# Attention on one Trainium2 core: the last 64 rows of q and k turned together, their scores by one tile over the whole array

## What is computed

```python
scores = scale * np.matmul(q, k.transpose(0, 1, 3, 2))          # scale = 1/8
cum = np.cumsum(np.maximum(s, 0.0), axis=-1)
bias = -(cum[:, :, :, None] - cum[:, :, None, :])
scores = np.where(causal, -1000000000.0, scores + np.minimum(bias, 0.0))
scores = scores - np.max(scores, axis=-1, keepdims=True)
attn = np.exp(scores); attn = attn / (np.sum(attn, axis=-1, keepdims=True) + 1e-09)
out = np.matmul(attn, v)
```

## Time and profile before

| what | value |
|---|---|
| median of 3 runs | 814.59 us (811.77 to 815.05) |
| profiled execution, its own time | 806.68 us |
| its span, first to last instruction | 804.9 us |
| TensorE matmul busy | 748.0 us (93%) |
| VectorE busy | 454.2 us (56%) |
| ScalarE busy | 284.5 us (35%) |
| GpSimd busy | 384.5 us (48%) |
| mean granted TensorE clock | 0.968 |
| attention, last product of TensorE | ends at about 223.4 us |

### The profile page before, as it was taken

The page is one execution under the profiler, slowest core; times in us unless marked ns, Lnnn a source line. Parts: engine busy times, 40 slices in busy tenths (PEclk is TensorE's granted clock), DMA queues, the critical chain, the costliest instruction groups (busy, mean ns, idle before and its releaser), DMA issues.

```text
span 804.9 us, 14992 instructions
## 1 busy us (share of the span) xinstructions
PE 748.0 (93%) x4920; PEld 613.1 (76%) x4920; DVE 454.2 (56%) x1018; ACT 284.5 (35%) x575; POOL 384.5 (48%) x468
## 2 busy tenths in 40 slices
PE   5999999999946999999999999998497999999998
PEld 2667777776735888888888888886397989979786
DVE  3667767667675444543544544443389962947800
ACT  3667776777520013111121221100154531524401
POOL 6557777777407549744444944400543521313300
PEclk9999999999966999999999999999598999999999
DMA  7787877766133575434433543000401111010011
GB/s 178 179 215 199 221 198 193 215 163 165 44 121 105 155 243 192 146 144 172 145 139 118 208 158 118 27 14 27 131 28 32 41 46 40 1 40 14 11 56 52
DMA packets 98055, 94.43 MB, mean 117 GB/s; under 512 B 62124, under 2 KB 71876, under 8 KB 97988
## 3 DMA queue, kind: packets, MB, share of 16 engines
q1 hardware_dynamic: 79748, 47.87, 21.7%
q10 hardware_dynamic: 14768, 34.38, 12.0%
q0 software_dynamic: 3472, 11.28, 4.7%
HBM read 77.44 MB, written 16.06 MB: 116 GB/s over the span
## 4 chain that ended last, share of the span: by engine, by line
PE 70%; DVE 14%; DMA 6%; POOL 4%; issue 3%; ACT 2%; SPq 1%; POOLq 0%; DVEq 0%; ACTq 0%
PE row_bank L1127 14%; PE wide_bank L1114 14%; PE row_bank L1306 8%; PE turn_ps L298 6%; PE score_ps L270 5%; DVE conv L1353 5%; PE turn_ps L395 5%; DMA x_slots<-x_rows,token_of 5%; PE wide_bank L1294 4%; DVE conv L1351 3%; PE turn_ps L356 3%; PE score_ps L264 2%; POOL ring L832 2%; PE wide_bank L1138 2%; PE turn_ps L275 2%
## 5 line engine op out<-in xcount | busy, mean ns | idle before, releaser
L832 POOL TENSOR_TENSOR ring<-raw_w,ring 128x2048 fp32r<-128x2048 f32 x30 | 137.7, 4613 | 85.7 <-ACT ring L822 85.7
L1114 PE MATMUL wide_bank<-ring,xs_tr 128*128 x600 | 145.8, 399 | 2.8 <-DVE xs_tr L1165 2.6
L1127 PE MATMUL row_bank<-ring,h_tr 128*128 x600 | 143.3, 394 | 1.9 <-DVE h_tr L1185 1.9
L822 ACT ACTIVATE ring<-raw_w 128x2048 fp32r<-128x2048 f32 x30 | 55.8, 1907 | 223.7 <-DMA raw_w<-in_moe_w_dram 194.4
L1114 PEld LDWEIGHTS wide_bank<-ring,xs_tr 128*128 128x128 f32 x600 | 112.9, 191 | 26.5 <-issue 3.7
L1127 PEld LDWEIGHTS row_bank<-ring,h_tr 128*128 128x128 f32 x600 | 110.9, 188 | 24.8 <-issue 2.1
L1294 PE MATMUL wide_bank<-x_tr,ring 128*128 128x288 f32 x768 | 109.8, 303 | 1.3 <-DVE x_tr L1327 1.3
L1294 PEld LDWEIGHTS wide_bank<-x_tr,ring 128*128 128x128 f32 x768 | 106.1, 194 | 2.1 <-DVE x_tr L1327 1.7
L1268 POOL TENSOR_TENSOR conv<-h_pad,conv 128x576 f32<-128x576 f32 x32 | 48.1, 1505 | 122.1 <-ACT conv L1378 122.0
L1306 PE MATMUL row_bank<-ring,g_tr 128*128 128x512 f32 x432 | 99.3, 390 | 3.0 <-ACT out_sb L1410 3.0
L1306 PEld LDWEIGHTS row_bank<-ring,g_tr 128*128 128x128 f32 x432 | 80.7, 188 | 20.7 <-DVE g_tr L1334 4.2
(11 more groups left out here) (176 smaller groups left out, 981.2 us busy)
## 6 DMA issues: line engine op xcount, KB each, us to landing
raw_w<-in_moe_w_dram ACTq DMA_DIRECT2D x12, 2048.0 KB, 10.1
ncum_row<-cum_rows SPq DMA_DIRECT2D x15, 576.0 KB, 4.1
y_sorted<-y_sb SPq DMA_DIRECT2D x25, 256.0 KB, 2.7
raw_w<-in_moe_w_dram SPq DMA_DIRECT2D x12, 512.0 KB, 3.9
ncum_tail<-cum_rows SPq DMA_DIRECT2D x32, 144.0 KB, 4.4
out_dram<-out_sb ACTq DMA_DIRECT2D x18, 256.0 KB, 2.0
q_nat<-in_q_dram SPq DMA_DIRECT2D x32, 128.0 KB, 3.9
v_nat<-in_v_dram SPq DMA_DIRECT2D x32, 128.0 KB, 2.4
```

Of the source, the lines that this page charges most:

```text
L832: nc.gpsimd.tensor_tensor(low, whole, high.bitcast(F32), ALU.subtract).then_inc(low_ready, 1)
L1114: last = nc.tensor.matmul(h_bank[:, half, :], xs_tr[:, a, kb, :], ring[:, bass.ds(n, 1), b, at:at + FH].rearrange("p a c -> p (a c)"), sta ...
L1127: last = nc.tensor.matmul(y_bank[:, :], h_tr[:, a, kb, :], ring[:, bass.ds(n, 1), 2 + b, kb * D:(kb + 1) * D].rearrange("p a c -> p (a c)" ...
```

## The change

`k_nat` loses its tail block; the k tail is loaded to partitions 64 to 127 of the tail block of `q_nat`, under the q tail. One transpose of the whole 128 x 128 tile then gives the turned q tail in 64 columns and the turned k tail in the next 64. `q_tail` becomes a tile of 128 x 128: its first 64 columns hold the q tail of the first head on that head's partitions and zeros elsewhere, its last 64 columns the same for the second head. VectorE writes it by one multiplication of the turned q tail, read twice, with a constant tile `own_head` (the scale on a head's own partitions, zero on the other's), which four memsets fill at the start. The tail scores are then two products (one for each half of the columns) of this tile with all 128 partitions of `k_tr`.

```diff
--- before.py
+++ after.py
@@ -53,7 +53,8 @@
     v_nat = [sb(f"v_nat{u}", [P, NT, 2 * D]) for u in range(2)]
     q_tr = [sb(f"q_tr{u}", [P, BODY]) for u in range(2)]
     k_tr = [sb(f"k_tr{u}", [P, S]) for u in range(2)]
-    q_tail = [sb(f"q_tail{u}", [P, TAIL]) for u in range(2)]
+    q_tail = [sb(f"q_tail{u}", [P, 2, TAIL]) for u in range(2)]
+    own_head = sb("own_head", [P, 2, TAIL])
     ncum_row = [sb(f"ncum_row{u}", [P, 2, S]) for u in range(2)]
     ncum_tail = [sb(f"ncum_tail{u}", [P, S]) for u in range(2)]
     ncum_diag_tail = sb("ncum_diag_tail", [P, TAIL])
@@ -74,7 +75,7 @@
     mask = sb("mask", [P, P])
     mask_tail = sb("mask_tail", [P, TAIL])
     q_nat = [sb(f"q_nat{u}", [P, NT, 2 * D]) for u in range(2)]
-    k_nat = [sb(f"k_nat{u}", [P, NT, 2 * D]) for u in range(2)]
+    k_nat = [sb(f"k_nat{u}", [P, FULL, 2 * D]) for u in range(2)]
 
     def over(name, shape, tensor):
         return nc.alloc_sbuf_tensor_at(name, shape, F32, offset=nc.lookup_mls(tensor).memorylocations[0].addr)
@@ -85,7 +86,7 @@
     score_ps = [ps(f"score_ps{n}", [P, 2, 512]) for n in range(2)]
     turn_ps = [ps(f"turn_ps{n}", [P, 512]) for n in range(4)]
 
-    consts_ready, masks_ready, zeros_ready = sem("consts_ready"), sem("masks_ready"), sem("zeros_ready")
+    consts_ready, masks_ready, zeros_ready, heads_ready = sem("consts_ready"), sem("masks_ready"), sem("zeros_ready"), sem("heads_ready")
     s_loaded, s_clipped, cum_ready, cum_stored = sem("s_loaded"), sem("s_clipped"), sem("cum_ready"), sem("cum_stored")
     col_turned, col_ready = sem("col_turned"), sem("col_ready")
     qk_loaded = [sem(f"qk_loaded{u}") for u in range(2)]
@@ -118,17 +119,17 @@
         return turn_ps[(13 * p + use) % 4]
 
     def sync_part(sp, early, between):
-        def load(dst, src, p, done, tail=0):
+        def load(dst, src, p, done, tail=0, tail_dst=None):
             heads = src[2 * p:2 * p + 2, :, :]
             for hh in range(2):
                 sp.dma_start(dst[:, 0:FULL, hh * D:hh * D + D], src[2 * p + hh, 0:BODY, :].rearrange("(i p) d -> p i d", p=P)).then_inc(done, 16)
-            sp.dma_start(dst[tail:tail + TAIL, FULL, :].rearrange("p (h d) -> p h d", h=2),
+            sp.dma_start((dst if tail_dst is None else tail_dst)[tail:tail + TAIL, FULL, :].rearrange("p (h d) -> p h d", h=2),
                          heads[:, BODY:S, :].rearrange("h p d -> p h d")).then_inc(done, 16)
 
         def load_qk(p):
             above(sp, k_turned, p - 1)
             load(q_nat[p % 2], q_h, p, qk_loaded[p % 2])
-            load(k_nat[p % 2], k_h, p, qk_loaded[p % 2])
+            load(k_nat[p % 2], k_h, p, qk_loaded[p % 2], tail=P - TAIL, tail_dst=q_nat[p % 2])
 
         def load_v(p):
             above(sp, pv_done, NT * (p - 1))
@@ -259,10 +260,8 @@
             above(pe, score_ready, unit(p, n - 2) if i else unit(p, 0) - 1)
             if i == FULL:
                 for half in range(2):
-                    for hh in range(2):
-                        at, rows = slice(hh * D, hh * D + D), slice(hh * TAIL, (hh + 1) * TAIL)
-                        last = nc.tensor.matmul(out[rows, half, 0:HALF], q_tail[u][at, :], k_tr[u][at, half * HALF:(half + 1) * HALF],
-                                                start=True, stop=True)
+                    last = nc.tensor.matmul(out[:, half, 0:HALF], q_tail[u][:, :, :].rearrange("p h c -> p (h c)"),
+                                            k_tr[u][:, half * HALF:(half + 1) * HALF], start=True, stop=True)
                 last.then_inc(scored, 1)
                 return
             for hh in range(2):
@@ -284,9 +283,7 @@
 
         def turn_qk_tails(p):
             u, bank = p % 2, turn(p - 1, 2)
-            nc.tensor.transpose(bank[:, 3 * P:3 * P + TAIL], q_nat[u][0:TAIL, FULL, :], identity[0:TAIL, 0:TAIL])
-            nc.tensor.transpose(bank[:, 3 * P + TAIL:4 * P], k_nat[u][0:TAIL, FULL, :], identity[0:TAIL, 0:TAIL])\
-                .then_inc(tails_turned, 1)
+            nc.tensor.transpose(bank[:, 3 * P:4 * P], q_nat[u][:, FULL, :], identity[:, :]).then_inc(tails_turned, 1)
 
         def turn_k(p):
             above(pe, out_moved, 2 * (p - 2) + 1)
@@ -472,6 +469,8 @@
         for hh in range(2):
             rows = slice(hh * TAIL, (hh + 1) * TAIL)
             nc.vector.tensor_copy(mask_tail[rows, :], mask[rows, rows]).then_inc(masks_ready, 1)
+            nc.vector.memset(own_head[rows, hh, :], SCALE)
+            nc.vector.memset(own_head[rows, 1 - hh, :], 0.0).then_inc(heads_ready, 1)
         dve.wait_ge(col_turned, 1)
         nc.vector.tensor_copy(cum_col[:, :, :], turn_ps[2][:, 0:FULL * HEADS].rearrange("p (i h) -> p i h", h=HEADS))\
             .then_inc(col_ready, 1)
@@ -513,7 +512,8 @@
         def move_qk_tails(p):
             u = p % 2
             dve.wait_ge(tails_turned, p + 1)
-            nc.vector.tensor_scalar(q_tail[u][:, :], turn(p - 1, 2)[:, 3 * P:3 * P + TAIL], SCALE, None, ALU.mult)
+            nc.vector.tensor_tensor(q_tail[u][:, :, :], turn(p - 1, 2)[:, 3 * P:3 * P + TAIL].unsqueeze(1).to_broadcast([P, 2, TAIL]),
+                                    own_head[:, :, :], ALU.mult)
             nc.vector.tensor_copy(k_tr[u][:, BODY:S], turn(p - 1, 2)[:, 3 * P + TAIL:4 * P]).then_inc(tails_moved, 1)
 
         def move_k(p):
@@ -584,6 +584,7 @@
 
         early(dve)
         dve.wait_ge(zeros_ready, 1)
+        dve.wait_ge(heads_ready, 2)
         move_qk_tails(0)
         move_k(0)
         add_bias(0, 0)
@@ -672,7 +673,7 @@
 
         for hh in range(2):
             act.dma_start(k_nat[0][:, 0:FULL, hh * D:hh * D + D], k_h[hh, 0:BODY, :].rearrange("(i p) d -> p i d", p=P)).then_inc(qk_loaded[0], 16)
-        act.dma_start(k_nat[0][0:TAIL, FULL, :].rearrange("p (h d) -> p h d", h=2), k_h[0:2, BODY:S, :].rearrange("h p d -> p h d"))\
+        act.dma_start(q_nat[0][P - TAIL:P, FULL, :].rearrange("p (h d) -> p h d", h=2), k_h[0:2, BODY:S, :].rearrange("h p d -> p h d"))\
             .then_inc(qk_loaded[0], 16)
         act.wait_ge(consts_ready, 4)
         nc.scalar.activation(gates[:, :, 0:P], identity[:, :].unsqueeze(1).to_broadcast([P, PER_B, P]), ACT.Copy).then_inc(gates_loaded, 1)
```

## The result

| | before | after |
|---|---|---|
| median, the runs of the result | 814.8 us (811.8 to 815.5, 4 runs) | 804.0 us (803.0 to 804.3, 4 runs) |
| ratio, 95% interval | | 0.987 (0.985 to 0.990) |
| profiled execution, own time / span | 806.7 / 804.9 us | 803.0 / 801.2 us |
| period of a pair | 12.85 us | 12.39 us |
| start of attention's last product | 221.83 us | 215.46 us |

What follows compares the result with a forecast made beforehand. TensorE was taken to bound attention. Tail scores (4.35 us) and turning the tails (2.31 us) sum to 6.7 us, so 814.6 - 6.7 = 807.9 us; range 805 to 811 within the forecast, 804 to 812.3 overall.

Steps and rivals of the forecast that it cites:

- attention's 6.7 us: Attention: tail scores save 15 x 0.29 = 4.35 us, turning the tails 14 x 0.165 = 2.31 us.
- TensorE bounds attention, and a pair's saving counts each time: Attention: TensorE is always busy, so its saving shortens every pair, the period going from 12.85 to 12.39 us.
- A change of shape costs 0.14 to 0.15 us, at two ends: TensorE in attention: entering the 128*128 shape costs 0.05 us extra, leaving it 0.09 us.
- Rival 3: Tail scores: the gaps belong to something else and return, so they save nothing; 812.3 us, chance 0.07.
- The whole-array slot goes by columns, 0.24 us: Tail scores: four whole-array slots of 288 columns take 0.24 us each, as the four slots before did.
- Rival 2: Tail scores: each pass waits for its own 0.19 us weight load; 4.8 us slower, 819.4 us, chance 0.03.
- The start doesn't gain: Attention's start: savings before 28.42 us only lengthen TensorE's 0.26 us wait for the k load of pair 2.
- VectorE hides the longer move: VectorE in attention: the multiplication takes 0.29 us, 0.08 more, hidden by 0.62 us idle ahead of L506.
- Rival 1: Attention: TensorE's freed time becomes a wait for ScalarE or VectorE, only turning the tails gains; 812.3 us, chance 0.08.
- The median: Whole kernel: the profiled execution's saving applies equally to the 814.6 us median, giving 807.9 us.
- the noise: Experts' start: when the clock rises can shift, for 1 or 2 us either way in both kernels.

Runs made afterwards that it cites:

- e2: Changed kernel with only the block-diagonal tail scores, tails loaded and turned as in the kernel before: 810.0 us, ratio 0.997 to the kernel before.
- e3: Changed kernel with only the tails' joined load and transpose, tail scores as in the kernel before: 812.6 us, ratio 1.000 to the kernel before.
- e8: Changed kernel with the two small 128*64 products moved next to the products with v: 801.5 us, ratio 0.986 to the kernel before.
- e5: Changed kernel with the tail scores in six products of 96 columns instead of two of 288: 813.0 us, one execution.
- e7: Changed kernel with SyncE's five small loads issued behind the loads of pair 2 instead of ahead: 799.1 us, one execution.
- e11: Changed kernel with the edits of e7, e8 and e9 together: 799.8 us, ratio 0.986 to the kernel before.
- e13: Changed kernel with the edits of e7 and e9, without that of e8: 798.9 us, ratio 0.986 to the kernel before.
- e12: Changed kernel with two more 128x512 sums on VectorE right behind the new multiplication: 799.4 us, one execution.
- e4: Changed kernel run again without an edit: 805.1 us, ratio 0.993 to the kernel before.
- e10: Changed kernel run again without an edit, on another chip than e4: 804.7 us, ratio 0.993 to the kernel before.
- e1: Kernel before, run again without an edit for a second trace: 814.4 us, beside 810.9 us in other runs of the same code.
- e9: Changed kernel with GpSimd's splitting of the third expert's weights put among the 25 gathers instead of behind them: 802.8 us, beside 804.7 unedited.

## Why the prediction was right

Direction and range held, the range by luck: the median of 804.02 us lies at its very end, 804. What the prediction worked out is attention's 6.7 us, and this was 6.4 by the logits' start; counted from the transposes of pair 2 on (28.42 and 28.69), it is 6.64. By its steps:

- **TensorE bounds attention, and a pair's saving counts each time.** Shown: the period went to the 12.39 us that was worked out, with no pair off it.
- **A change of shape costs 0.14 to 0.15 us, at two ends.** Shown by e2 (0.30 for two), e3 (0.16 for one and a little array time), and e8, where two more went from other instructions. Rival 3 (it doesn't do what it says) is out.
- **The whole-array slot goes by columns, 0.24 us.** Shown: four slots in 0.97. Rival 2 (loads in the open) is out at this length, and e5 shows from where a load decides: slots under 0.109 us. The 0.19 us that the rival took for a load is too much for one that follows another.
- **The start doesn't gain.** Right, and by 0.27 us worse in this trace, through a later landing, which differs by more than that between executions. That load, not TensorE, sets the start: with it issued first (e7, e11, e13) the wait is gone, and the transposes start at 27.40 to 27.79.
- **VectorE hides the longer move.** Right: the multiplication took 0.27 us (0.29 forecast). But I had looked for its cover at the wrong place. The idle time before L505 is 0.33, which is 0.62 - 0.29 with nothing taken off for the multiplication: that came out of the idle time before L500. By e12 the cover is at least 1.26 us, where the two idle times make 1.05: here they were a lower bound of the cover, not the cover.
- **Rival 1 (the freed time becomes a wait)** didn't come about for this change, and did for the next one of its kind, e8.
- **The median.** I took 814.6 as where the kernel before stands. Its timed executions on five occasions (84, with the outliers 818.9 and 822.9 left out: 805.7 to 817.9) have a median of 811.9, those of the changed kernel on three (28, 799.7 to 811.3) one of 804.3; the fastest are 6.0 us apart. The interval of the result (8 to 12.5 us) leaves the forecast out, those of e4 and e10 (about 2.5 to 9 us) hold it. So the 10.8 us of the result are 6.4 us of attention, and beyond that the draw: three of the four executions of the kernel before were long ones. The term that was mis-sized is the noise, put at 1 or 2 us. Its main source in the traces is the wait for the third expert's weights, 0 to 5.3 us, with the clock's dip behind it (1.6 us more in e1, 2.4 in e10), and I had not looked for what sets it, though the 7.9 us between the profiled execution and the median called for it. That the long executions of untraced runs are of the same kind is likely, and only argued; e9 and e13, where they are missing, speak for it.
- **The 2.6 us given back.** TensorE's timeline near the end of the experts, in the first trace before and in the first after:

```profile
556.27 5.73 PE L1127 MATMUL row_bank<-ring,h_tr 128*128 x24 [1.91 <-DVE h_tr L1185]
569.11 1.09 PE L1276 MATMUL bank<-identity,y_tok 128*128 128x128 f32 x4 [7.11 <-DVE y_tok L1321]
```

```profile
550.10 7.37 PE L1128 MATMUL row_bank<-ring,h_tr 128*128 x24 [1.92 <-DVE h_tr L1186]
564.62 1.08 PE L1277 MATMUL bank<-identity,y_tok 128*128 128x128 f32 x4 [7.15 <-DVE y_tok L1322]
```

The changed kernel is 6.2 us ahead at the first of these rows, 4.5 at the second, 4.0 at 587 us and 3.7 at the end: the run of 24 records took 1.6 us longer. The stage around it, each kernel in its own time (columns of the earlier trace rows), before, after, and in e1, which is the kernel before:

```profile
545.00:565.00 20.00, 15.09 (x70) 12.06 (x68) 5.15 (x8) 0.00 (x0) 0.00 (x0) 1.00 0.08 27
```

```profile
540.00:560.00 20.00, 15.56 (x65) 12.23 (x63) 4.47 (x7) 0.00 (x0) 0.00 (x0) 0.91 0.07 27
```

```profile
550.00:570.00 20.00, 16.20 (x68) 12.83 (x66) 5.03 (x8) 0.00 (x0) 0.00 (x0) 0.91 0.04 15
```

The clock dips to 0.91 in the trace after and not in the one before; but it does so in e1 too, where nothing was changed. So most of what was given back is a dip that the kernel before has as well in some executions. Of the changed kernel's traces e4 and e10 have it too, and among its variants e7, e8, e12 and e13 don't; which executions have it is open. The other 1 us is not accounted for.

## What to carry to other kernels

Read TensorE's timeline from start to start, with the shape of the tile beside each run, and solve for the slot and for what is left over at each change of shape. Where small products stand among whole-array ones, a block-diagonal tile that keeps the shape can be cheaper than concurrent small tiles, although half of it multiplies zeros. Prove such a small gain by the period in the trace and not by medians, which differed by 3.5 us for one and the same code. And where a profiled execution and the median of the runs lie apart, look for a wait that some executions draw and others don't, before anything is forecast in us.

## What the runs showed of the hardware

- On 128*128 tiles, in float32, at a granted clock of 1.00, a slot is the longer of two: 0.109 us for a load of 128 columns (e5), and the columns streamed, 0.24 us for 288.
- A change of tile shape cost 0.09 us ahead of the new shape's first record and 0.05 us in its first slot, the same to 0.01 or 0.02 us for 64*128, 128*64 and 64*64 against 128*128, for products and transposes alike (e2, e8). The weight loads of the changed kernel show something beside it:

```profile
144.17 0.42 PEld L295 LDWEIGHTS turn_ps<-identity,prob 128*128 128x128 f32 x4 [0.17 <-issue]
144.56 0.79 PEld L263 LDWEIGHTS score_ps<-k_tr,q_tail 128*128 128x128 f32 x4
```

  The load behind the change of shape starts with its own transpose (TensorE's row: 144.18), the one inside the shape 0.11 us ahead of its product (144.67). Whether this late load is what the change costs is not shown.
- A wait of TensorE of 3 to 5 us in the middle of dense work was followed by a stretch at 1.2 GHz, 3.6 to 6.8 us long by the granted clock (0.91 in e1, 0.83 in e10, over 20 us): 1.6 and 2.4 us on top of the wait, by the run behind it. Behind a wait of 1.9 or 2.0 us near the experts' end such a dip came in some executions (after, e1, e4, e10) and not in others (before, e7, e12, e13), for 1.6 us.
